# Weight pieces, ranking and tile 1's gather moved at the seam to the experts

## What is computed

```python
x = softmax(q @ mean8(k).T / 8) @ mean8(v)            # 8 heads of 64
a = x @ w1;  b = x @ w2                               # 512 -> 1024
x = (a * b @ w3) @ w_out                              # 1024 -> 512
logits = x @ w_gate + modality_bias[modality_id]      # 8 experts
e_idx = argmax(logits, axis=1)
gate_w = softmax(logits)[n, e_idx]
for e in range(8):
    mask = e_idx == e
    h = np.maximum(x[mask] @ e_w1[e], 0.0)
    out[mask] = gate_w[mask, None] * (h @ e_w2[e])
```

## Time and profile before

| | us |
|---|---|
| median of 3 runs | 1263.77 |
| lowest, highest | 1261.28, 1264.49 |
| the profiled execution, its own time | 1261.98 |
| its span, first to last instruction | 1260.1 |

### The profile page before, as it was taken

The page is one execution under the profiler, slowest core; times in us unless marked ns, Lnnn a source line. Parts: engine busy times, 40 slices in busy tenths (PEclk is TensorE's granted clock), DMA queues, the critical chain, the costliest instruction groups (busy, mean ns, idle before and its releaser), DMA issues.

```text
span 1260.1 us, 29770 instructions
## 1 busy us (share of the span) xinstructions
PE 1182.2 (94%) x12126; PEld 1109.2 (88%) x12127; DVE 647.0 (51%) x1219; ACT 394.4 (31%) x906; POOL 422.2 (34%) x394
## 2 busy tenths in 40 slices
PE   8778999889999899999999999889999999999996
PEld 7667988889898798999999999779989989989996
DVE  0477797877979685563454456622222234222221
ACT  1265454445445443232322233111111122111111
POOL 2843667656666654542000001022112112112111
PEclk9888999999999999999999999989999999999998
DMA  9831635536363533225455456043111111111111
GB/s 351 270 114 55 172 114 152 151 91 175 90 181 109 139 85 99 95 66 168 129 136 140 128 136 225 10 144 108 51 37 53 43 33 49 36 42 58 33 42 42
DMA packets 99890, 137.12 MB, mean 109 GB/s; under 512 B 16835, under 2 KB 66115, under 8 KB 99780
## 3 DMA queue, kind: packets, MB, share of 16 engines
q1 hardware_dynamic: 40340, 78.77, 21.0%
q10 hardware_dynamic: 53040, 36.29, 10.1%
q0 software_dynamic: 6400, 20.50, 5.2%
HBM read 92.99 MB, written 43.06 MB: 108 GB/s over the span
## 4 chain that ended last, share of the span: by engine, by line
PE 51%; DMA 2%; DVE 1%; issue 1%; ACT 0%; POOL 0%; POOLq 0%; ACTq 0%; DVEq 0%
PE ab L731 6%; PE ab L733 6%; PE ab L732 6%; PE x2p L731 5%; PE x2p L732 5%; PE x2p L733 5%; PE rt L731 5%; PE rt L733 5%; PE rt L732 5%; PE sct L901 1%; DMA x_rows<-xr 1%; DMA out<-y_out,tok_c 0%; PE ab L892 0%; DMA xg<-x_rows,idx_c 0%; DVE gl L1452 0%
## 5 line engine op out<-in xcount | busy, mean ns | idle before, releaser
L731 PE MATMUL ab<-xth,e1h 128*128 128x256 f32 x608 | 172.9, 284 | 4.0 <-DVE acc L1547 4.0
L732 PE MATMUL ab<-xtl,e1h 128*128 128x256 f32 x608 | 172.6, 284 | 0.0
L733 PE MATMUL ab<-xth,e1l 128*128 128x256 f32 x608 | 172.6, 284 | 0.0
L1332 ACT ACTIVATE hth<-ab 128x512 fp32r<-128x512 f32 x76 | 45.4, 597 | 341.4 <-PE ab L733 328.7
L710 POOL DMA_INDIRECT out<-y_out,tok_c x38 | 38.5, 1012 | 327.9 <-DVE y_out L1871 327.3
L1850 DVE SCALAR_TENSOR_TENSOR htl<-ab,hth 128x512 fp32r<-128x512 f32 x76 | 52.4, 691 | 164.1 <-ACT hth L1332 164.1
L731 PEld LDWEIGHTS ab<-xth,e1h 128*128 128x128 f32 x608 | 117.3, 193 | 4.9 <-DVE acc L1547 4.2
L732 PEld LDWEIGHTS ab<-xtl,e1h 128*128 128x128 f32 x608 | 117.3, 193 | 0.7
L733 PEld LDWEIGHTS ab<-xth,e1l 128*128 128x128 f32 x608 | 117.2, 193 | 0.0
L731 PE MATMUL x2p<-xh,wh 128*128 128x256 f32 x336 | 99.5, 296 | 8.7 <-DVE xl L1418 7.6
L731 PE MATMUL ab<-xh,wh 128*128 128x256 f32 x336 | 98.3, 293 | 9.8 <-DVE xl L1418 9.6
(11 more groups left out here) (227 smaller groups left out, 3391.3 us busy)
## 6 DMA issues: line engine op xcount, KB each, us to landing
gr<-g_rows SPq DMA_DIRECT2D x36, 512.0 KB, 4.5
kv<-in_v SPq DMA_DIRECT2D x24, 512.0 KB, 3.7
qt<-in_q ACTq DMA_DIRECT2D x38, 256.0 KB, 2.8
kv<-in_k SPq DMA_DIRECT2D x16, 576.0 KB, 6.1
g_rows<-gst ACTq DMA_DIRECT2D x72, 128.0 KB, 2.1
g_rows<-gst ACTq DMA_DIRECT2D x36, 256.0 KB, 2.8
x_rows<-xr SPq DMA_DIRECT2D x36, 256.0 KB, 4.0
stage<-in_moe_w SPq DMA_DIRECT2D x8, 1024.0 KB, 8.2
```

The lines of the kernel that those rows point to most:

```text
L731: pe.matmul(outp, lh, rh, start=first, stop=False)
L732: pe.matmul(outp, lh, rl, start=False, stop=False)
L733: return pe.matmul(outp, ll, rh, start=False, stop=last)
L1332: act.activation(hth[:, 2 * n:2 * n + 2, :].rearrange("p f n -> p (f n)"), ab[n // 2][:, n % 2, :], ACT.Relu).then_inc(hth_ready, 1)
```

## The change

1. The four weight pieces are no longer issued together ahead of the store of group 30's rows. One is issued behind the row store of each of the groups 30 to 33 (`FIRST_PIECE = NG - 6`), on the same SP queue, the first of them also behind `load_g(35)`.
2. `PIECE_AT`: ACT splits piece 2 after the second half of group 33 (before: the first half of group 34) and piece 3 after the second half of group 34 (before: the first half of group 35).
3. `gh3` moves up by 128 bytes, so that it no longer overlaps with tile 0's half of `xg`. The first gather waits for groups up to 31 (before: up to 33). Because `gh3` now reaches into the next block of `wh`, `load_g` of groups 1 to 4 waits for one product of the first stage more.
4. Block 7's rank and tables lie in `ab4[:, 3]`; the wait of TensorE for their addition moves from ahead of `mul_h(0)` to ahead of its part f = 6.
5. Block 8's rank moves from behind f = 4 to behind f = 1, its tables 0 and 1 behind f = 4, 2 and 3 behind f = 7. DVE's order follows: one-hots 0 and 1 ahead of the first `htl`, the decode ahead of the last.
6. DVE itself copies tile 1's two index columns behind the decode (the column number is still in a register), and POOL gathers tile 1 on this, ahead of its wait for the step tables.

```diff
-PIECE_AT = {0: 0, 2: 1, 4: 2, 6: 3}
+PIECE_AT = {0: 0, 2: 1, 3: 2, 5: 3}
+FIRST_PIECE = NG - 6
-        gh = [at(f"gh{n}", hi_at[n] * KB, [P, FC, P], F32R) for n in range(RING)]
+        gh = [at(f"gh{n}", hi_at[n] * KB + (P if n == 3 else 0), [P, FC, P], F32R) for n in range(RING)]
-            return rt if b == B else ab4[:, 0, :]
+            return rt if b == B else ab4[:, 3 if b == B - 1 else 0, :]
...
-                    sp.wait_ge(prod_done[(t - 1) // 2], POS * STAGES)
+                    sp.wait_ge(prod_done[(t + 1) // 2], POS * STAGES)
...
-                if b == B - 1 and g == 2:
-                    sp.wait_ge(first_ready, 1)
-                    e = sp.value_load(first_i[0:1, 0:1], min_val=0, max_val=E - 1)
-                    for c in range(4):
-                        load_piece(e, c)
                 sp.wait_ge(xr_ready, 2 * (t + 1))
                 sp.dma_start(x_rows[P * t:P * (t + 1), 0:DM], xr[:, g % 2, 0:DM]).then_inc(x_stored[g % 2], 16)
                 if t + RING < NG:
                     load_g(t + RING)
+                if t == FIRST_PIECE:
+                    sp.wait_ge(first_ready, 1)
+                    e = sp.value_load(first_i[0:1, 0:1], min_val=0, max_val=E - 1)
+                if FIRST_PIECE <= t < FIRST_PIECE + 4:
+                    load_piece(e, t - FIRST_PIECE)
...
-            pool.wait_ge(x2_done, 2 * (NG - 2))
+            pool.wait_ge(x2_done, 2 * (NG - 4))
...
-            pool.wait_ge(rows_ready, 1)
             for half in range(2):
                 pool.wait_ge(x_stored[half], 16 * (G // 2) * STAGES)
             pool.wait_ge(meta_stored, 16 * STAGES)
+            pool.wait_ge(idx_copied, 1)
+            for n in range(2, 4):
+                pool.indirect_dma_start(
+                    out=xg[:, n, :], out_offset=None, in_=x_rows,
+                    in_offset=bass.IndirectOffsetOnAxis(ap=idx_c[:, n:n + 1], axis=0)).then_inc(
+                        gathered[n], 16)
...
             pool.wait_ge(index_ready, 1)
-            gather(1, 1)
             step(0, 0, 0, True)
...
             def after_h(f):
+                if f == 1:
+                    rank(B)
                 if f == 4:
-                    rank(B)
+                    table(B, 0)
+                    table(B, 1)
+                if f == 5:
+                    pe.wait_ge(acc_added, B)
                 if f == 7:
-                    table(B, 0)
+                    table(B, 2)
+                    table(B, 3)
 
             def after_y(half, f):
-                if half == 0 and f < G - 1:
-                    table(B, f + 1)
                 if half and f == 4:
                     turn_x(1, 1, 1)
 
-            pe.wait_ge(acc_added, B)
...
+                dve.wait_ge(rows_ready, 1)
+                dve.tensor_copy(idx_c[:, 2:4], acc[:, bass.ds(first_at + 2, 2)]).then_inc(idx_copied, 1)
...
             route_gate(B)
-            lo_ht(0, [0])
             route_rank(B)
             route_onehot(B, 0)
             route_onehot(B, 1)
-            lo_ht(0, [1, 2])
+            lo_ht(0, [0])
             for g in range(2, G):
                 route_onehot(B, g)
+            lo_ht(0, [1, 2])
+            decode()
             lo_ht(0, [3])
-            decode()
             step_tables()
```

More of the change, by code:

```diff
@@ L1735, in first_rows @@
                                          op0=ALU.add, op1=ALU.add).then_inc(index0_ready, 1)
+                return col
             for b in range(STAGES):
@@ L1769, in group @@
                     if b == B - 1:
-                        first_rows()
+                        return first_rows()
             for t in range(NG):
-                group(t // G, t % G)
+                col = group(t // G, t % G)
+                if t == G * B - 1:
+                    first_at = col
             def decode():
```

## The result

The changed kernel takes 1244.89 us (median; 1242.17 to 1245.84), the kernel before 1262.53 in the same timing (1259.59 to 1264.49): ratio 0.9844, interval 0.9812 to 0.9876. It is 17.6 us faster, where 15.5 were forecast. Two later timings gave 1245.8 (0.9864, 0.9842 to 0.9886) and, in five rounds, 1247.08 (0.988, 0.9858 to 0.9901). The profiled execution of the changed kernel took 1244.21 us, its span is 1242.5.

A forecast was written before the change was run, and what follows sets the result against it. TensorE, busy 94% of the span, was taken as the bound, so only its waits and lower clock count. Gains 0.9 + 5.4 + 8.9 = 15.2, corrected to 15.5, gave 1263.77 - 15.5 = 1248.3 us, range 1245.0 to 1255.0.

The forecast's parts named there:

- Term 1: Second MLP: with group 30's store ahead of the weight pieces, TensorE's 0.87 us wait for the `xr` copy goes; gain 0.9.
- no row for `xr`: Sign in the changed kernel's TensorE waits: the 0.87 us wait for the copy of `xr` no longer appears.
- Term 2: Start of tile 0: piece 3 split sooner and L1547's addition awaited later remove the 3.96 us idle and lower clock; gain 5.4.
- one alone I put at the lower end: Piece 3, sent singly, lands at the low end of 5.1 to 11.2 us: issued about 778.5, landed 783.6.
- if ACT waits for piece 3 past 785: Sign ahead of tile 0 that would make the forecast wrong; piece 3 was expected landed at 783.6.
- rival B: Tile 0's start: piece 3 lands after 11.2 us, 6.0 us lost with the clock, total 1254.3; chance 0.11.
- Ranking and tables, cost 0: Tile 0's first product: last block's ranking and one-hot tables fit in with slack 0.8 and 0.6; at worst a few tenths.
- Term 3: Tile 1's rows: gathers straight after the decode land at 811.0, TensorE asks at 811.8, the wait goes; gain 8.9.
- Rival A: Tile 1's gather slowed by 2.1 us beside DVE's `htl` and tiny operations: 1.3 us wait, total 1249.6 to 1251; chance 0.17.
- The sum: Whole kernel: 0.9 + 5.4 + 8.9 = 15.2, corrected to 15.5 us gained; 1263.77 - 15.5 = 1248.3.
- C: Both gathers held back to their old times, little gain left: 1260 to 1263, no measurable difference; chance 0.05.
- D: Slower than before: single pieces land late, TensorE stands until the last is split; decides from about 20 us landing; chance 0.03.

The follow-up runs named there:

- the run with the gather behind the tables: Changed kernel with tile 1's gathers again only behind the step tables, without DVE's early index copy: 1250.28 us, ratio 0.9898 to the kernel before.
- both runs with later pieces: Changed kernel with each weight piece asked for one group later: 1263.79 us (1.0008); the same with ACT's and DVE's splits one group later too: 1253.38 us (0.9933).
- the run with the old ranking: Changed kernel with block 8's ranking and tables where the kernel before had them on DVE: 1246.89 us, ratio 0.9869.
- the filled kernel: Kernel before with unused matmuls put into TensorE's two long waits, ahead of tile 0's product and tile 1's transposes: 1258.92 us, ratio 0.9973.

## Where the prediction was right, and which steps failed

**Term 1, `xr`, 0.9.** Right in the trace that it was set against, and only in part as a rule. The sign "no row for `xr`" holds in the changed kernel's first trace; its two later ones have 0.6 us, and the run with the gather behind the tables 0.3. In those three the copy waits behind piece 2's split and no longer for a store. The size was one sample too: the four traces with four pieces in a row show 0.9 to 2.4.

**Term 2, tile 0's start, 5.4.** The two causes were the right ones. The step that failed is "one alone I put at the lower end": piece 3 was asked for at 778.1 on the scale of the trace before (775.00 and the 3.11 us that this trace is ahead), as forecast (778.5), but landed after 7.7 us and not 5.1. The 5.1 was no price for this place: it is the fastest of the four loads at 843 us, and at the seam itself none of the trace before landed in under 6.9. Single pieces that overlap with the one before by 1.5 us at most (both runs with later pieces) land in 6.4 to 6.8 here. Piece 3 of the changed kernel was asked for 2.7 us before piece 2 had landed; that this overlap makes the rest of its 7.7 is likely and not tested. By the prediction's own sign, "if ACT waits for piece 3 past 785", the step failed: 782.73 is 785.8 on the old scale. The slack of 1.2 us became a wait of 1.13, 0.28 and 0.43 in three traces, 0.6 us of `xr` beside the latter two; rival B had the mechanism, and its landing in full (11.2) did not come. Sending the pieces one group sooner removes the wait. The rest of the term, 1.4 for the clock, was read from one trace. The same wait cost 2.7 in the second and, by its first layer, 2.3 in a third: it is a sample, too, and the low side of it.

**Ranking and tables, cost 0.** `oh` was ready at 790.09, TensorE asked at 791.20; the second pair of one-hots at 795.10, asked at 795.67. Slack 1.1 and 0.6 against 0.8 and 0.6 forecast. DVE took 3.65 us between them, as forecast.

**Term 3, tile 1's rows, 8.9.** Right. The second gather was issued at 805.22, 808.3 on the old scale, for 807.4 forecast; the transposes began at 809.40 with no wait. The second layer is 9.3 and 10.0 us shorter, for 8.9 and its half of the 0.3. `xtl` of tile 1 was not late: TensorE's first product of tile 1 came 3.10 us after its transposes with no idle ahead of it. Rival A foresaw a slow issue beside DVE's `htl` and the small operations. The issues took 0.94 and 0.95 us; they lay beside the step tables only, so `htl` stays untested. What slows an issue the traces do show. In all fifteen a gather of tile 0 was issued while DVE was at a subtraction with two inputs in SBUF, and its issue ended 0.8 to 1.05 us after that, whatever was left of it: in the trace before the split ends at 783.17 and the 3.04 us of the earlier trace rows at 783.99, in the changed kernel `gl` ends at 765.43 (below) and the 1.87 us at 766.45.

```profile
764.21 1.22 DVE L1460 TENSOR_TENSOR gl<-gr,gh 128x1024 fp32r<-128x1024 f32 x1
```

So GpSimd stood until DVE's operation was over, and then needed its usual 0.95. The Trainium skill's rule on the shared ports (SBUF — State Buffer, "Who interferes with whom") has a second half that the prediction left out: its two-port modes leave out tensor_tensor, but one with both inputs in SBUF contends with a GpSimd instruction that reads SBUF. For the writing of descriptors the section counts such an operation out, by inference, and there the measurement decides. The gather reads its indices in SBUF, and the rows agree with the second half; the one-hots, to which the prediction gave a share, are not needed for it.

**The sum.** 15.5 forecast, less the 1.13 of waiting left, makes 14.4; the seams give 14.5 against the profiled run it was made on. By the second trace of before it is 16.6, by the timings 17.6, 16.9 and 15.7. So sign, place and size were right, and the forecast failed on what it was set against and on its range. The result lies 3.4 us below the forecast. Of these 1.2 are the start: 1263.77 was a median of three, and the same timing with one run more gave 1262.53; 15 to 19 runs later gave 1262.6 to 1262.8, though twelve of the kernel before again gave 1264.11. The other 2.1 are gain beyond 15.5, where the seams show 1.0 less to 1.1 more. The low end was put 3.3 us below the forecast, with 2 us for scatter and nothing for a larger gain, though the clock's part had been read from a single stretch of 14 matmuls (1.4, measured 1.3 to 2.7) and the wait for `xr` from a single row (0.9, measured 0.9 to 2.4). Both have a long side, and it is the side of more gain. Beyond that it was chance: the two later timings, 1245.8 and 1247.08, lie inside the range, and a median of four runs between 1242.17 and 1245.84 does not fix 0.11 us. Nor is all of the nearness merit: the late piece made the gain 1.1 us smaller than forecast, the dearer clock up to 1.3 larger, and the two work against each other.

**Rivals.** C fell with the first wait list. D, the loss, was priced wrongly: "each microsecond beyond 6.3 us from issue costs one", deciding from about 20 us to land. One for one holds only as long as a piece's request doesn't stand behind the split of the piece before. With the ring closed, a delay of one group (some 6 us) costs 17 us, at landings of only 6.4 us. The slowest landing at this seam was 8.3 us in the changed kernel (769.44 to 777.73) and 8.9 in its trace of five rounds, so the other way into D, 20 us to land, did not come near.

## What to carry to other kernels

When loads are spread between the steps of a loop, draw the ring: load, its consumer on an in-order engine, what stands behind the consumer there, the store behind that, and the next load behind the store; it must span more steps than a load takes, and in this kernel one step of distance was the difference between 17 us gained and none. A load sent singly still lands in the traffic of its neighbours, so take its time from loads at the same place and not from the fastest row of the whole trace. A wait's price in clock is a sample like any other: take it from several traces, or fill the wait once and time it.

## What the hardware showed that was not expected

- After the same idle of 3.96 us TensorE ran 14 matmuls at the lower level in one trace and 27 in another, 1.4 and 2.7 us; a third (3.98 us) lay between, at 2.3. With the waits filled, the granted clock stayed at 1.00 and the whole kernel took 3.7 us less with more work in it.
- A wait of 1.13 us, and one of 1.15 in the run with the old ranking, left the granted clock at 1.00. One of 2.39 us, in the filled kernel, was followed by 0.87 over 13 us.
- A GpSimd gather issued while DVE subtracts two tensors in SBUF is held until DVE has finished: 1.87 to 3.07 us instead of 0.95, in fifteen traces.
- The fastest of the loads of 1 MB took 7.5 to 7.7 us in three traces of the changed kernel and 6.4 in both runs with later pieces. The Trainium skill, in DMA: Bandwidth & Descriptors, section "Anatomy of one DMA — SWDGE (gpsimd) path", fits 2.0 us and bytes by 436 GB/s to a DMA issued by GpSimd, an estimate of 4.4 us for 1 MB; these are SP's, and no load of `stage` here landed in under 5.1.
